# Last chunk's expert logits with the expert vectors as weights, and its ranks behind the first expert tile

## What is computed

```python
# attention: B=4, H=8, S=768, D=64; x is then (3072, 512)
state = gamma * state + k[t] v[t]^T ;  y[t] = scale * q[t] state
# MLP: 512 -> 2048 -> 512
h = x @ w_in
x = (max(h, 0) + alpha * min(h, 0)) @ w_out
# experts: E=8, 512 -> 1024 -> 512
xn = x / (norm(x) + 1e-6) ;  en = expert_emb / (norm(expert_emb) + 1e-6)
logits = xn @ en.T / tau
expert_idx = argmax(logits, axis=1)
gate_w = softmax(logits)[expert_idx]
out[token] = gate_w * (max(x @ w1[e], 0) @ w2[e])
```

## Time and profile before

| | us |
|---|---|
| median of 3 runs | 951.67 |
| lowest, highest | 951.37, 951.69 |
| profiled execution, whole | 952.91 |
| its span, first to last instruction | 950.8 |
| TensorE busy in the span | 937.3 |
| VectorE busy | 653.4 |
| ScalarE busy | 305.1 |
| GpSimd busy | 253.9 |

### The profile page before, as it was taken

One profiled execution on the slowest core, in us unless ns is written; L12 is line 12 of the kernel. 1 busy time (PEld: TensorE's weight loads), 2 busy tenths in 40 slices (PEclk: granted clock), 3 DMA queues, 4 the chain that ended last, 5 costly groups with the idle time before them and its releaser, 6 DMA issues.

```text
span 950.8 us, 16235 instructions
## 1 busy us (share of the span) xinstructions
PE 937.3 (99%) x5700; PEld 798.2 (84%) x5700; DVE 653.4 (69%) x1150; ACT 305.1 (32%) x419; POOL 253.9 (27%) x192
## 2 busy tenths in 40 slices
PE   8999999999999999999999999999999999999996
PEld 7888888888888888888888888899999999878885
DVE  5656589747984698559965897776755557799641
ACT  4232121112111121112111222235555557677541
POOL 4453214341434144413433122520000001100101
PEclk9999999999999999999999999999999999999998
DMA  8432297024001500140002302179866667799611
GB/s 308 155 117 78 92 392 239 1 89 145 0 0 44 188 0 0 44 156 10 1 24 78 122 1 89 45 290 331 316 229 230 227 225 274 297 358 357 230 42 55
DMA packets 32754, 139.76 MB, mean 147 GB/s; under 512 B 5264, under 2 KB 5648, under 8 KB 23970
## 3 DMA queue, kind: packets, MB, share of 16 engines
q1 hardware_dynamic: 25186, 120.51, 35.0%
q0 software_dynamic: 4336, 12.61, 3.4%
q10 hardware_dynamic: 3168, 5.79, 1.9%
HBM read 126.27 MB, written 28.41 MB: 163 GB/s over the span
## 4 chain that ended last, share of the span: by engine, by line
PE 96%; DMA 2%; DVE 1%; issue 0%; SPq 0%; ACT 0%; POOL 0%; POOLq 0%; ACTq 0%; DVEq 0%
PE bank L761 28%; PE bank L779 27%; PE bank L914 15%; PE bank L876 10%; PE bank L854 6%; PE bank L656 2%; PE bank L700 2%; PE bank L672 2%; PE bank L746 1%; PE bank L689 1%; PE bank L891 1%; DMA attention<-in_w_exp 1%; DMA attention<-in_qk 1%; PE bank L725 0%; DVE weights_split L1271 0%
## 5 line engine op out<-in xcount | busy, mean ns | idle before, releaser
L761 PE MATMUL bank<-activations_split,weights_split 128*128 128x512 f32 x1152 | 277.6, 391 | 0.0
L779 PE MATMUL bank<-weights_split,activations_split 128*128 128x512 f32 x1152 | 276.0, 389 | 0.0
L779 PEld LDWEIGHTS bank<-weights_split,activations_split 128*128 128x128 f32 x1152 | 216.1, 188 | 44.8
L761 PEld LDWEIGHTS bank<-activations_split,weights_split 128*128 128x128 f32 x1152 | 215.2, 188 | 45.8 <-issue 1.1
L1806 POOL TENSOR_TENSOR activations_split<-scratch,activations_split 128x512 fp32r<-128x512 f32 x84 | 123.7, 1472 | 304.4 <-ACT activations_split L1551 299.7
L1551 ACT CAST activations_split<-scratch 128x512 fp32r<-128x512 f32 x96 | 59.8, 623 | 411.5 <-DVE scratch L1050 411.5
L914 PE MATMUL bank<-weights_split,activations_split 128*128 128x512 f32 (+1 forms) x648 | 158.2, 396 | 0.0
L914 PEld LDWEIGHTS bank<-weights_split,activations_split 128*128 128x128 f32 x648 | 118.5, 188 | 23.2
L1045 DVE TENSOR_SCALAR scratch<-bank,alpha 128x512 f32<-128x512 f32 x96 | 71.7, 747 | 93.7 <-PE bank L761 93.2
L1271 DVE TENSOR_TENSOR weights_split<-attention,weights_split 128x2048 fp32r<-128x2048 f32 (+1 forms) x45 | 102.4, 2289 | 25.9 <-ACT weights_split L1631 25.7
L1864 POOL DMA_INDIRECT out<-scratch,y_token x27 | 32.6, 1206 | 276.1 <-ACT scratch L1664 276.1
(11 more groups left out here) (245 smaller groups left out, 741.8 us busy)
## 6 DMA issues: line engine op xcount, KB each, us to landing
attention<-in_w_exp SPq DMA_DIRECT2D x48, 1024.0 KB, 5.8
en_all<-in_w_exp SPq DMA_DIRECT2D x16, 1024.0 KB, 7.2
attention<-in_kv SPq DMA_DIRECT2D x43, 256.0 KB, 4.2
expert_rows<-in_pad_rows SPq DMA_DIRECT2D x8, 1285.0 KB, 25.1
rows<-in_w_mlp SPq DMA_DIRECT2D x14, 512.0 KB, 3.4
attention<-in_qk SPq DMA_DIRECT2D x12, 512.0 KB, 5.4
rows<-expert_rows ACTq DMA_DIRECT2D x22, 257.0 KB, 2.9
scratch<-in_qk SPq DMA_DIRECT2D x10, 512.0 KB, 3.9
```

Source lines behind the costliest of these rows:

```text
L761: last = mm(H_ps[f % 2][:, :], win(a, kc, f), x[:, kc, :], start=(k == 0), stop=(k == 3 * KC - 1))
L779: last = mm(bank[j][:, :], x[f % 2][:, j * P:(j + 1) * P], wout(a, f), start=(f == 0 and a == 0 and part_ == "hi"), stop=(f == FB - 1 and ...
```

## The change

The normalised expert vectors are kept in two parts (`en_hi`, `en_lo`), side by side as 16 columns. In the last chunk ScalarE writes the turned rows as float32r high parts and VectorE the low parts, into the half of the weight buffer that the second pair's expert fills later. `last_logits` is one call behind the second hidden group: the 16 expert columns are the weights, 512 turned rows move, and high and low rows are added up in one PSUM tile of 16 by 512. ScalarE copies it to SBUF; `logits_turned` turns it back with four small transposes behind the third hidden group, and `router_choose` adds the two halves before it goes on.

VectorE's list is written in another order: the low part of the first hidden group directly after the choice of pairs, the second ahead of the norms, the others ahead of the choice and of the gate, and `router_place` behind the first weight quarter of the second expert and the low part of tile 2. TensorE's count and rank matmuls stand behind the first expert tile. ScalarE's exponentials stand behind the fourth high part.

```diff
+    en_two = sb("en_two", KC * 2 * E, f32r)[:, :].rearrange("p (k e) -> p k e", k=KC)
+    en_hi, en_lo = en_two[:, :, 0:E], en_two[:, :, E:2 * E]
...
+    LT_ps, lt_sb = bank[7], EN[0:2 * E, 0:TB]
+    LG_ps = bank[6][:, 0:B * 2 * E].rearrange("p (b e) -> p b e", b=B)
...
-            def last_logits(j):
-                pe.wait_ge(s_xt, due(s_xt, j + 1))
+            def last_logits():
+                pe.wait_ge(s_xt, due(s_xt, B))
                 for kc in range(KC):
-                    last = mm(LG_ps[:, j, :], last_xT(j)[:, kc * P:(kc + 1) * P], enT[:, kc, :],
-                              start=(kc == 0), stop=(kc == KC - 1))
+                    if kc == KC - 1:
+                        pe.wait_ge(s_xtl, due(s_xtl, B))
+                        for n in range(KC):
+                            mm(LT_ps[0:2 * E, :], en_two[:, n, :], last_lo[:, n], start=False, stop=False)
+                    last = mm(LT_ps[0:2 * E, :], en_two[:, kc, :], last_hi[:, kc], start=(kc == 0), stop=(kc == KC - 1))
+                last.then_inc(s_LT, 1)
+
+            def logits_turned():
+                pe.wait_ge(s_lt, due(s_lt, 1))
+                for j in range(B):
+                    last = tr(LG_ps[:, j, :], lt_sb[:, j * P:(j + 1) * P], ident[0:2 * E, 0:2 * E])
                 last.then_inc(s_R2, 1)
...
-            up_two(0, 1, between=last_logits)
+            up_two(0, 1)
+            last_logits()
             up_two(0, 2)
-            router_rank(NC - 1)
-            mm(CNT_ps, ones, seen[:, :, B], start=True, stop=True).then_inc(s_cnt, 1)
+            logits_turned()
             up_two(0, 3)
...
-            expert_down(0, 0, None, between=lambda: x_transpose(0, 2))
+            def logits_read_then_transpose():
+                pe.wait_ge(s_lsum, due(s_lsum, 2))
+                x_transpose(0, 2)
+
+            expert_down(0, 0, None, between=logits_read_then_transpose)
+            pe.wait_ge(s_oh, due(s_oh, NC))
+            mm(CNT_ps, ones, seen[:, :, B], start=True, stop=True).then_inc(s_cnt, 1)
+            router_rank(NC - 1)
...
-                link(ve.tensor_tensor(L, logits, bc(inv, E), ALU.mult))
+                    ve.tensor_copy(L2, logits[:, :, 0:E]).then_inc(s_lsum, 1)
+                    dve.wait_ge(s_lsum, due(s_lsum, 1))
+                    ve.tensor_tensor(L2, L2, logits[:, :, E:2 * E], ALU.add).then_inc(s_lsum, 1)
+                    dve.wait_ge(s_lsum, due(s_lsum, 2))
+                link(ve.tensor_tensor(L, L2, bc(inv, E), ALU.mult))
...
-            ve.tensor_copy(enT, EMB_ps)
+            ve.tensor_copy(en_hi, EMB_ps).then_inc(s_en2, 1)
+            dve.wait_ge(s_en2, due(s_en2, 1))
+            ve.tensor_tensor(en_lo, EMB_ps, en_hi.bitcast(f32), ALU.subtract)
...
             choose_pairs()
+            h_two_low(0, 0)
+            for j in range(B):
+                dve.wait_ge(s_xt, due(s_xt, j + 1))
+                ve.tensor_tensor(last_part(1, j), last_ps(j)[:, :], last_part(0, j).bitcast(f32), ALU.subtract).then_inc(s_xtl, 1)
...
+            h_two_low(0, 1)
             router_norm(NC - 1)
-            h_two_low(0, 0)
+            h_two_low(0, 2)
             router_choose(NC - 1, LG_ps)
-            h_two_low(0, 1)
+            h_two_low(0, 3)
             router_gate(NC - 1)
-            router_place(NC - 1)
-            h_two_low(0, 2)
-            h_two_low(0, 3)
             split_expert(1, (0,))
             x_lo_part(2, 2)
+            router_place(NC - 1)
             split_expert(1, (1,))
...
-                se.copy(last_xT(j), last_ps(j)[:, :]).then_inc(s_xt, 1)
+                se.copy(last_part(0, j), last_ps(j)[:, :]).then_inc(s_xt, 1)
...
-            exps(NC - 1)
+            act.wait_ge(s_LT, due(s_LT, 1))
+            se.copy(lt_sb, LT_ps[0:2 * E, :]).then_inc(s_lt, 1)
             h_two_high(0, 2)
             h_two_high(0, 3)
+            exps(NC - 1)
```

More of the change, by code:

```diff
@@ L223, in build @@
     tau_in, tau_sb = sb("tau_in", 1, f32), sb("tau", 1, f32)
-    enT = sb("enT", KC * E, f32)[:, :].rearrange("p (k e) -> p k e", k=KC)
+    en_two = sb("en_two", KC * 2 * E, f32r)[:, :].rearrange("p (k e) -> p k e", k=KC)
+    en_hi, en_lo = en_two[:, :, 0:E], en_two[:, :, E:2 * E]
     emb_ss, emb_nrm, emb_inv, emb_half = (sb(n, 1, f32) for n in ("emb_ss", "emb_nrm", "emb_inv", "emb_half"))
@@ L299, in Y_of @@
         return Y_first[hp] if isinstance(c, int) and c == 0 else Y_ps[hp % 2]
-    LG_ps = bank[7][:, 0:B * E].rearrange("p (b e) -> p b e", b=B)
+    LT_ps, lt_sb = bank[7], EN[0:2 * E, 0:TB]
+    LG_ps = bank[6][:, 0:B * 2 * E].rearrange("p (b e) -> p b e", b=B)
     RK_ps = bank[6][:, 0:B * E].rearrange("p (b e) -> p b e", b=B)
-    RK_last = bank[3][:, 0:B * E].rearrange("p (b e) -> p b e", b=B)
+    RK_last = bank[7][:, 0:B * E].rearrange("p (b e) -> p b e", b=B)
     CNT_first, CNT_ps = bank[6][:, 64:64 + E], bank[7][:, 64:64 + E]
@@ L332, in build @@
     s_emb_ld, s_en_st, s_en_all, s_en_last = sem("emb_ld"), sem("en_st"), sem("en_all"), sem("en_last")
+    s_LT, s_lt, s_xtl, s_lsum, s_en2 = sem("LT"), sem("lt"), sem("xtl"), sem("lsum"), sem("en2")
     s_star, s_tail, s_fill = sem("star"), sem("tail"), sem("fill")
@@ L388, in last_ps, with last_part @@
         return bank[j]
-    def last_xT(j):
-        return Y[:, j * TB:(j + 1) * TB]
+    def last_part(a, j):
+        return W[:, HALF + (a * B + j) * DM:HALF + (a * B + j + 1) * DM]
+    last_hi, last_lo = (W[:, HALF + a * B * DM:HALF + (a + 1) * B * DM].rearrange("p (j k c) -> p k j c", j=B, k=KC)
+                        for a in range(2))
     def bc(ap, n):
@@ L858, in up, with up_two @@
                 last.then_inc(s_M1, 1)
-            def up_two(i, g, between=None):
+            def up_two(i, g):
                 slot = i % 2 * HALF
@@ L879, in up_two @@
                             k += 1
-                        if between is not None and kc % 2 and (j, kc) != (1, KC - 1):
-                            between(2 * j + kc // 2)
                 last.then_inc(s_M1, 1)
-                if between is not None:
-                    between(3)
             def h_transpose(t):
@@ L900, in expert_down @@
                     pe.wait_ge(s_yd, due(s_yd, t - 1))
-                elif isinstance(t, int) and t == 1:
-                    pe.wait_ge(s_rk, due(s_rk, NC))
                 k = 0
@@ L1127, in router_choose @@
                 else:
-                    dve.wait_ge(s_R2, due(s_R2, 4))
-                link(ve.tensor_tensor(L, logits, bc(inv, E), ALU.mult))
+                    dve.wait_ge(s_R2, due(s_R2, 1))
+                    ve.tensor_copy(L2, logits[:, :, 0:E]).then_inc(s_lsum, 1)
[3 more added lines that the diff above has]
+                link(ve.tensor_tensor(L, L2, bc(inv, E), ALU.mult))
                 link(ve.tensor_reduce(top, L, AX, ALU.max))
```

## The result

The changed kernel takes 955.16 us in the median of 12 runs (954.11 to 958.28), the kernel before 951.68 beside it: a ratio of 1.004, 95% interval 1.003 to 1.005. It is slower by 3.5 us, where the prediction had +1.0 and a range up to 954.8. Its profiled execution has a span of 953.8, 3.0 above the one of before.

The account below looks back on a forecast made before the run. TensorE, at 96% of the span, was taken to bound the kernel. Saving 1.27, adding 0.2 at the head and 2.1 of waiting gave +1.0 on the 951.67 median: 952.7 us, range 950.4 to 954.8.

Parts of the forecast that it names:

- the wait: TensorE, before the fourth hidden group of the third pair: idle for a late W2 half, 2.1 us (1.1 to 3.6).
- the fourth scatter's landing: GpSimd's fourth scatter of the last chunk's rows: lands 5.5 us after its start, at 648.5 (647.4 to 649.9).
- What TensorE saves: TensorE, second hidden group and last chunk's logits: 5.05 us of work replaces 6.32, 1.27 us saved.
- The head: Normalised expert vectors, near 107.8: a second VectorE step that needs the first adds 0.2 us.
- What moves: slot_i ends 7.6 us later, at 637.1, delaying scatters, row loads and the third pair's first W2 half, landing at 671.4.
- "slower" rival: Fourth scatter lands 6.9 to 8.8 us after its start; wait 3.5 to 5.4, time 954.1 to 956.0; chance 0.19.
- Doubled matmuls: Rival: the 8 logits matmuls with 16 weight columns cost double, 3.66 us; time 954.5; chance 0.03.
- covers: TensorE would not wait for VectorE's low parts (covered by 1 us) or at tile 2's transpose (some 3 us).

## Why the prediction was wrong

The forecast named the place and the mechanism of the wait. One term of its sum was too small, the fourth scatter's landing (5.5, measured 6.6), and with it the wait (2.1, measured 2.86). Another was missing, the slower work behind the wait (nothing, measured 1.54).

- **What TensorE saves: right.** Logits 1.85 against 1.83, turning back 0.35 against 0.34. The whole stretch saved 1.07 and not 1.27, because the fourth hidden group took 3.08 and the rank and tile pieces a little more than the rows of before gave them.
- **The head: right.** The chain has 0.20 for the new copy with the step that waits for it, and the reciprocal starts at 108.05 in place of 107.82: +0.23. The chain there in the changed kernel:

```profile
107.72 0.20 DVE en_two L1261
...
107.94 0.04 DVE en_two L1263
...
108.05 0.17 DVE tau L1264
```

- **What moves: right until the scatters land.** slot_i ended at 636.95 (forecast 637.1); the first scatter was held by VectorE's split and took 2.16 (forecast 2.2). By the inference of the Trainium skill, SBUF — State Buffer, Who interferes with whom, that such an instruction does not stop descriptor generation, the scatter would not have been held. It was: in all thirteen profiles every scatter of this chunk that began inside a two-input split took 2.16 to 2.86 in place of 0.96 to 0.98, and ended 0.8 to 0.9 behind the split. A scatter also reads slot_i, so the runs do not tell whether that reading or the descriptor generation was stopped.
- **The fourth scatter's landing: the first term that was mis-sized.** I took 5.5 us, between a quiet and a busy row. It landed after 6.6, and after 6.1 to 7.1 in the ten other profiles of kernels with the ranks moved or the placing late. So the row loads went out at 650.26 and not 649.3, the W2 half at 662.91, and its landing (9.1, forecast 9.3) made the wait 2.86 and not 2.1. This is the "slower" rival, whose landing of 6.4 was passed. Its reason can be seen in part: the weight load issued at 639.31 took 97.5% of the DMA engines' time between 642 and 644 and 26.7% between 644 and 646. The forecast held that nothing follows it; but GpSimd's two output scatters were issued at 644.10 and 645.40, and its queue took 99.6% and 96.8% between 646 and 648. Which of the two made the landing late is not shown. With this wait alone the time would have been 951.68 - 1.07 + 0.23 + 2.86 = 953.7, inside the stated range.
- **The clock after the wait: the term that was missing.** I priced the wait as a gap and took all work behind it at the full clock and at once at its usual pace. The 1.54 us (1.28 for the clock, 0.26 for starting again) are larger than the whole saving of the change, and the run with the filled wait shows that they come from idling. With 2.86 and 1.54 in place of 2.1 the sum is -1.07 + 0.23 + 2.86 + 1.54 = +3.56; the medians differ by 3.48. That these agree to a tenth is partly luck, since the profiled spans differ by 3.0.
- **Doubled matmuls, and covers.** Wide float32r matmuls with 16 weight columns are not doubled, and the low parts and tile 2's transpose made nobody wait, as said.

What stays open: why some waits of about 2 us leave the clock up (1.67 and 2.06) and others do not (2.31 and 2.86); four profiles are too few to say more than that. The DMA traffic does not sort them: in the wait of 1.67 it was as heavy as in the two long ones (share 0.99 to 1.03), in that of 2.06 there was none (0.00). Also open is what held ScalarE ahead of the wait of 0.81 at 653 in the run with the late placing alone, and which traffic made the fourth scatter land late.

## What to carry to other kernels

When a step is moved, follow its result through every queue to the last load that stands behind it: here a 0.9 us step on VectorE, moved by 7.5, delayed a weight load over four queues by 6.4, of which all but 2.86 was hidden. A transfer that nobody needs soon (the padding) does not belong ahead of one with a date, nor a wait for it ahead of the next loads. And a wait on TensorE is to be priced with the work behind it: here 0.26 for starting again after any wait, and after the two longest (2.31 and 2.86) 1.5 and 1.3 more for the lower clock.

## What the runs showed of the hardware

TensorE's granted clock fell from 2.4 to 1.2 GHz in two profiles in which it had stood idle for 2.31 and 2.86 us, in the first of them only 0.7 us after it had begun again, and it was back some 3 us later; the group of 24 matmuls behind cost 1.50 and 1.28 more than after a wait at full clock. After 0.81, 1.67 and 2.06 us idle it did not fall (each time 3.14 for the group, 0.26 above its usual 2.88), and with the gap filled by matmuls whose result nobody reads it stayed up. A float32r matmul of 512 columns costs 0.23 with 16 weight columns as with 128. An indirect DMA of GpSimd that begins inside a VectorE instruction of 2.29 us with two SBUF inputs ends only 0.8 to 0.9 us after that instruction, in all thirteen profiles. The same DMA of 128 rows lands 2.9 to 8.8 us after its start in the kernel before (24 of them, 3.4 in the median), and 6.1 to 7.1 for the fourth one of the last chunk where it was sent late.
